# Another order of gatings, low parts and down products in a fused attention and feed-forward kernel

## The reference, cut to what matters

```python
xn = x / sqrt(mean(x * x) + 1e-6) * rms_g          # first layer
g = xn @ w_gate                                     # 512 -> 1536
val = xn @ w_val                                    # 512 -> 1536
x1 = (g * sigmoid(g) * val) @ w_out                 # 1536 -> 512
h = x1 @ w_in                                       # second layer, 512 -> 2048
y = (h * sigmoid(h)) @ w2_out                       # 2048 -> 512
```

## Time and profile before

| what | value |
|---|---|
| time, median of 3 (lowest to highest) | 916.54 us (915.85 to 919.73) |
| the profiled execution: time, span in the trace | 915.6 us, 913.9 us |
| mean granted clock of TensorE | 0.994 |
| busy: TensorE, VectorE, ScalarE, GpSimd | 884.3, 520.3, 343.7, 254.3 us |
| chain that ended last: TensorE, issue, GpSimd, VectorE | 85%, 4%, 4%, 4% of the span |

### The profile page before, as it was taken

How to read it: one execution, slowest core, us unless ns; L and a number is a source line. 1 busy time by engine, 2 the same in 40 slices (tenths; PEclk the granted TensorE clock), 3 DMA queues, 4 the chain that set the end, 5 groups by cost and what they waited for, 6 DMA issues and landing times.

```text
span 913.9 us, 12772 instructions
## 1 busy us (share of the span) xinstructions
PE 884.3 (97%) x4902; PEld 831.2 (91%) x4902; DVE 520.3 (57%) x865; ACT 343.7 (38%) x668; POOL 254.3 (28%) x266
## 2 busy tenths in 40 slices
PE   4898998999999999999999999999999999999998
PEld 4787898999999999999999999999999898889897
DVE  7788863777654666655655445666545544343433
ACT  2576844444222232354554232232233332332222
POOL 2776378888200000547775100000000000000000
PEclk9999998999999999999999999999999999999999
DMA  9843355776875555166759666555554545474321
GB/s 272 223 127 107 114 218 219 276 277 267 341 278 208 207 207 208 43 257 227 291 214 391 241 236 250 205 209 208 206 191 174 207 173 207 173 271 177 127 89 74
DMA packets 55724, 191.67 MB, mean 210 GB/s; under 512 B 21872, under 2 KB 32112, under 8 KB 42608
## 3 DMA queue, kind: packets, MB, share of 16 engines
q1 hardware_dynamic: 55664, 190.85, 58.0%
HBM read 134.74 MB, written 56.10 MB: 209 GB/s over the span
## 4 chain that ended last, share of the span: by engine, by line
PE 85%; issue 4%; POOL 4%; DVE 4%; DMA 2%; SPq 1%; ACT 1%; POOLq 0%; DVEq 0%; ACTq 0%
PE ps L1218 15%; PE ps L1219 14%; PE ps L1220 14%; PE ps L1282 7%; PE ps L1283 7%; PE ps L1281 7%; PE ps L1255 6%; PE ps L1256 6%; PE ps L1257 5%; PE ps L1152 1%; DMA qs<-in_q 1%; DVE al L990 1%; PE ps L1124 1%; DVE vt L983 1%; POOL rstd L568 1%
## 5 line engine op out<-in xcount | busy, mean ns | idle before, releaser
L1218 PE MATMUL ps<-xh,wr 128*128 128x384 f32 x840 | 282.6, 336 | 3.8 <-DVE qt L956 1.6
L1220 PE MATMUL ps<-xh,wr 128*128 128x384 f32 x840 | 281.1, 335 | 0.0
L1219 PE MATMUL ps<-xl,wr 128*128 128x384 f32 x840 | 280.9, 334 | 0.0
L1218 PEld LDWEIGHTS ps<-xh,wr 128*128 128x128 f32 x840 | 157.7, 188 | 8.3 <-DVE qt L956 2.5
L1219 PEld LDWEIGHTS ps<-xl,wr 128*128 128x128 f32 x840 | 157.7, 188 | 0.9
L1220 PEld LDWEIGHTS ps<-xh,wr 128*128 128x128 f32 x840 | 157.7, 188 | 0.0
L1283 PE MATMUL ps<-wo,al 128*128 128x512 f32 x288 | 112.5, 391 | 0.0
L1282 PE MATMUL ps<-wo,ah 128*128 128x512 f32 x288 | 112.4, 390 | 0.0
L1281 PE MATMUL ps<-wo,ah 128*128 128x512 f32 x288 | 112.0, 389 | 0.0
L1003 DVE TENSOR_TENSOR xacc<-ps,xacc 128x384 f32<-128x384 f32 (+1 forms) x102 | 62.4, 612 | 70.0 <-PE ps L1257 39.2
L1255 PE MATMUL ps<-ah,wo 128*128 128x384 f32 x288 | 97.8, 340 | 3.4 <-ACT qt L685 3.1
(11 more groups left out here) (128 smaller groups left out, 1171.8 us busy)
## 6 DMA issues: line engine op xcount, KB each, us to landing
wr<-ring_home SPq DMA_DIRECT2D x40, 1792.0 KB, 7.3
ring_home<-wr SPq DMA_DIRECT2D x20, 1792.0 KB, 8.1
wo<-out_home SPq DMA_DIRECT2D x28, 1024.0 KB, 4.8
out_home<-wo SPq DMA_DIRECT2D x14, 1024.0 KB, 9.6
raw_c<-in_moe_w_out SPq DMA_DIRECT2D x13, 512.0 KB, 7.3
qs<-in_q SPq DMA_DIRECT2D x16, 256.0 KB, 4.0
kv<-in_k SPq DMA_DIRECT2D x3, 1024.0 KB, 7.1
kv<-in_v SPq DMA_DIRECT2D x3, 1024.0 KB, 8.6
```

The costliest lines, as they stand in the source:

```text
L1218: pe.matmul(out_ps, w_hi, x_hi, start=first and c == 0, stop=False, skip_group_check=True)
L1219: pe.matmul(out_ps, w_hi, x_lo, start=False, stop=False, skip_group_check=True)
L1220: ins = pe.matmul(out_ps, w_lo, x_hi, start=False, stop=c == 1, skip_group_check=True)
```

## The change

Five edits, all in order and waits; no operation is added or left out.

1. The gatings have an order of their own, C11, C21, C12, C22, and the high and low parts of the first layer follow it. In the V unit run the first three gatings and low part 0, behind them; the gating of C22 runs in the following unit, between combine_u2 and combine_u3, and low parts 1, 2 and 3 after combine_u3. ScalarE makes one high part in the V unit and three in the following one.
2. A down of the first layer takes its products in the order perm 0, perm 1, rot 0, rot 1, perm 2, rot 2, rot 3, perm 3. It starts when two low parts are there and waits for all four at rot 0.
3. copy_down of a phase's last down moves out of that down's place in ScalarE's list into the unit behind it, after keep_first and the high parts. For the last down of all it stays.
4. In a down of the first layer the first of the token parts due there runs ahead of the first addition of a rot.
5. The waits follow: the overwriting of qt by keep_first, combine_u2 and combine_u3 waits for the gating that reads the same block, and banks BY and BZ are free after the second and third gating.

```diff
--- before.py
+++ after.py
@@ -113,10 +113,11 @@
                 (BX, 1, 1, False), (BY, 2, 6, False), (BZ, 6, 2, False)]
     C11, C12, C21, C22 = 0, 1, 2, 3
     SILUS = [C11, C22, C21, C12]
-    SPLITS = {1: [C11, C22, C21, C12], 2: [C11, C21, C22, C12]}
-
-
-    DOWN1 = [("rot", 0), ("rot", 1), ("perm", 0), ("perm", 1), ("rot", 2), ("rot", 3), ("perm", 2), ("perm", 3)]
+    GATES = [C11, C21, C12, C22]
+    SPLITS = {1: GATES, 2: [C11, C21, C22, C12]}
+
+
+    DOWN1 = [("perm", 0), ("perm", 1), ("rot", 0), ("rot", 1), ("perm", 2), ("rot", 2), ("rot", 3), ("perm", 3)]
     ROTBANK = [BR, BX, BR, BX]
 
 
@@ -660,7 +661,7 @@
                 if units[u][1] == "V":
                     gated = [m for m in range(n) if ffn_of[m] == 1]
                     if gated:
-                        act.wait_ge(s_lo, 4 * gated[-1] + 3)
+                        act.wait_ge(s_lo, 4 * gated[-1] + 2)
                     if downs[n] == (3, 0):
                         act.wait_ge(s_wlo, len(made))
                     if n == 0:
@@ -669,7 +670,7 @@
                     act.wait_ge(s_vb, B)
                     act.wait_ge(s_kTm, B)
                 elif ffn_of[n - 1] == 1:
-                    act.wait_ge(s_hd, hd0[n - 1] + 3)
+                    act.wait_ge(s_hd, hd0[n - 1] + 2)
                 else:
                     act.wait_ge(s_lo, 4 * (n - 1) + 2)
                 act.activation(tiles(u)[:, C21, :], ps[:, BX, 0:BLOCK], ACT.Copy).then_inc(s_snap, 1)
@@ -732,8 +733,12 @@
                     squares(NT - 1)
                     norm(NT - 1)
                 if prior == 1:
+                    high(n - 1, 1)
                     high(n - 1, 2)
                     high(n - 1, 3)
+                prev = before["unit", x]
+                if prev and prev[0] == "down" and prev[1] in last_down:
+                    copy_down(prev[1])
                 if x in (1, 2):
                     weight_high(made_at["r", x + 1] - (x == 2))
                 if x == 2:
@@ -750,7 +755,6 @@
                     weight_high(made_at["o", N2 + g])
                 if letter == "V":
                     high(n, 0)
-                    high(n, 1)
                 else:
                     silu(x, 0)
                     silu(x, 1)
@@ -810,8 +814,6 @@
                 if ph < 5:
                     for f in HIGH_AT[PHASES[ph][0]].get(g, ()):
                         token_high(ph + 1, f)
-                if x in last_down:
-                    copy_down(x)
                 if letter == "I":
                     high(n, 0)
                     high(n, 1)
@@ -948,7 +950,7 @@
                 if units[u][1] == "V" and gated:
                     dve.wait_ge(s_lo, 4 * gated[-1] + 4)
                 elif units[u][1] != "V" and n and ffn_of[n - 1] == 1:
-                    dve.wait_ge(s_hd, hd0[n])
+                    dve.wait_ge(s_hd, hd0[n - 1] + 3)
                 elif units[u][1] != "V" and n:
                     dve.wait_ge(s_lo, 4 * n)
                 dve.wait_ge(s_prod, NF * u + 2)
@@ -957,6 +959,9 @@
                    .then_inc(s_c, 1)
 
             def combine_u3(u):
+                n = units[u][3]
+                if units[u][1] != "V" and n and ffn_of[n - 1] == 1:
+                    dve.wait_ge(s_hd, hd0[n])
                 dve.wait_ge(s_prod, NF * u + 4)
                 dve.tensor_tensor(tiles(u)[:, C22, :], ps[:, BY, 0:BLOCK], tiles(u)[:, C21, :], ALU.add)\
                    .then_inc(s_c, 1)
@@ -973,12 +978,12 @@
                    .then_inc(s_c, 1)
 
             def gate(u, i):
-                n, c = units[u][3], SILUS[i]
-                dve.wait_ge(s_silu, 4 * n + i + 1)
+                n, c = units[u][3], GATES[i]
+                dve.wait_ge(s_silu, 4 * n + SILUS.index(c) + 1)
                 if c == C11:
                     dve.wait_ge(s_prod, NF * u + 5)
                 else:
-                    dve.wait_ge(s_c, 5 * u + 2 + i)
+                    dve.wait_ge(s_c, 5 * u + 2 + SILUS.index(c))
                 value = vt[:, c, :] if c == C22 else ps[:, {C11: BX, C21: BY, C12: BZ}[c], 0:BLOCK]
                 dve.tensor_tensor(vt[:, c, :], qt[:, c, :], value, ALU.mult).then_inc(s_hd, 1)
 
@@ -1012,21 +1017,21 @@
                 if x == 0:
                     scale_x(NT - 2)
                 if prior == 1:
-                    low(n - 1, 0)
-                    low(n - 1, 1)
+                    gate(x - 1, 3)
                 combine_u3(x)
                 if prior == 1:
+                    low(n - 1, 1)
                     low(n - 1, 2)
                     low(n - 1, 3)
                 if letter == "V":
                     gate(x, 0)
-                    gate(x, 1)
                 combine_last(x, C21)
                 if letter == "V":
-                    gate(x, 2)
+                    gate(x, 1)
                 combine_last(x, C12)
                 if letter == "V":
-                    gate(x, 3)
+                    gate(x, 2)
+                    low(n, 0)
 
             sum_keys(0, 0)
             dve.wait_ge(s_frontsum[0], 1)
@@ -1075,6 +1080,10 @@
                     letter = None
                     low(x, 2)
                     low(x, 3)
+                if ffn_of[x] == 1:
+                    for i in todo[:1]:
+                        token_part(ph + 1, i)
+                    todo = todo[1:]
                 add_down(x, 0)
                 add_down(x, 1)
                 for i in todo[:-1]:
@@ -1191,7 +1200,7 @@
                 elif i == 1 and u == 0:
                     pe.wait_ge(s_shift, NT)
                 elif i in (1, 2) and u and units[u - 1][1] == "V":
-                    pe.wait_ge(s_hd, hd0[units[u - 1][3]] + 2 + i)
+                    pe.wait_ge(s_hd, hd0[units[u - 1][3]] + 1 + i)
                 elif i in (1, 2) and u:
                     pe.wait_ge(s_c, 5 * u - 2 + i)
                 elif i == 3:
@@ -1235,8 +1244,10 @@
                 ph, g = downs[n]
                 w, ends = wo[o_slot(n)], (g == 0, g == GROUPS[1] - 1)
                 weights_of_down(n)
-                pe.wait_ge(s_lo, 4 * n + 4)
+                pe.wait_ge(s_lo, 4 * n + 2)
                 for kind, m in DOWN1:
+                    if kind == "rot" and m == 0:
+                        pe.wait_ge(s_lo, 4 * n + 4)
                     if kind == "rot" and m == 0 and n == 0:
                         pe.wait_ge(s_xc, NT)
                     elif kind == "rot" and m == 0:
```

## The result

| | before | changed |
|---|---|---|
| median of 6 runs (lowest to highest) | 916.53 us (915.85 to 919.73) | 909.34 us (907.92 to 912.24) |
| the profiled execution: time, span, mean granted clock | 915.6, 913.9, 0.994 | 909.0, 907.3, 0.998 |
| start of unit 0 in the trace | 111.71 us | 110.35 us |

The ratio is 0.9926 [0.9904, 0.9949]: 7.2 us faster, where 2.9 was forecast and 909.8 was the low end of the range.

What follows compares the result with a forecast made beforehand. TensorE was taken as the bound, busy 884.3 of 913.9 us, so only its waits could be won. Terms 0.5 + 0.35 + 2.0 + 0.86 + 0.4 - 1.2 = 2.9 us gave 913.6 us, range 909.8 to 917.3.

Steps and rivals of the forecast that it cites:

- First down: First layer's first down: silu chain 1.57 us late, five products left behind the wait instead of seven; gain 0.5 us.
- Unit 4: Unit 4: old stall at product 5 goes, product 3 stalls 0.7 us behind weight copies; gain 0.35 us.
- Units 6, 8, 10 and the down starts: Gating of C22 out of the V unit ends stalls at product 1, leaving 0.25 us each; gain 2.0 us.
- Rots later: Rots later in first-layer downs: banks free in time, slack 0.28 us; cost 0, at most 0.1 in each of 18.
- Unit 53: Unit 53, behind a phase's last down: copies of standing outputs moved a unit later remove its stall; gain 0.86 us.
- unit 45: Unit 45, behind a phase's last down: only the copy ahead of high 0 goes; gain 0.4 us.
- Unit 25: Unit 25: later load puts GpSimd's sums over the four low parts, 1.05 us each, not 0.47; loss 1.2 us.
- the lock of the earlier trace: VectorE and GpSimd on SBUF: VectorE's operation ends some 0.42 us after GpSimd's current one; GpSimd's next loses about 0.33.
- Weights pacing phase 0: Rival: TensorE waits again for GpSimd's weights for what it gains in phase 0; no gain, 916.5 us; chance 0.14.
- The clock was down for half as long: Rival on the first down: shorter wait keeps the clock at 2.4 GHz, 2.6 us more, 911.0 us; chance 0.12.
- No collisions: Rival: GpSimd's operations fall beside the moved ones in units 4 to 10 and 25; gain 6.1, 910.4 us; chance 0.17.
- The lock costing more than it gave: Rival: waits on GpSimd cost 2.0 us in each of units 4, 6, 8, 10; slower, 920.1 us; chance 0.09.

Runs made afterwards that it cites:

- experiment 5: The changed kernel as it is, in more executions: 912.71 us (8 runs), ratio 0.9959 against the kernel before.
- run 7: The kernel before with only ScalarE's copy of the first output weights moved from unit 2 into unit 1: 908.93 us, ratio 0.9930.
- run 6: The changed kernel with ScalarE's copy of the first output weights moved from unit 2 into unit 1: 905.47 us, ratio 0.9889 against the kernel before.
- run 2: The changed kernel with the copies of the standing outputs back in the last down's place: 913.31 us, ratio 0.9977 against the kernel before.
- run 3: The kernel before with only the down's new product order, its wait for three low parts and the token part moved ahead: 913.73 us, ratio 0.9976.
- run 4: The changed kernel with the old order of the down's products, all four low parts awaited at its start: 916.92 us, ratio 1.0016 against the kernel before.
- run 1: The kernel before with only the copies of the standing outputs moved a unit later: 914.61 us, ratio 0.9993.
- Run 8: The changed kernel with the raw tile's load in unit 24 also waiting for the second addition of down 11: 912.24 us, one execution.
- run 9: Changed kernel, first output weights' copy in unit 1, unit 3's high 0 ahead of its weight copies, second output weights' copy in unit 4: 905.77 us, ratio 0.9896.
- run 10: The changed kernel with low part 0 in the following unit, ahead of the moved gating: 912.59 us, one execution.

## Why the prediction was wrong

Point by point, in the order of the prediction.

**First down: +0.5, measured +1.54.** The chain came where it was put. The timeline of the changed kernel, from the copy to the product that waits:

```profile
130.35 1.04 ACT L622 ACTIVATE wo<-raw_f 128x1024 fp32r<-128x1024 f32 x1
...
131.47 1.29 POOL L552 TENSOR_TENSOR wo<-raw_f,wo 128x512 fp32r<-128x512 f32 x1 [5.13 <-ACT wo L622]
...
132.73 1.60 POOL L553 TENSOR_TENSOR wo<-raw_f,wo 128x512 fp32r<-128x512 f32 x1
...
137.12 0.73 POOL L533 TENSOR_TENSOR wt<-raw_g,wt 128x256 f32<-128x256 f32 x1
...
139.74 0.47 ACT L686 ACTIVATE qt<-ps 128x384 f32<-128x384 f32 x1
...
140.26 0.69 PE L1266 MATMUL ps<-ah,wo 128*128 128x384 f32 x1 [2.46 <-ACT qt L686]
```

Unit 2 began 1.67 us earlier than before (126.40, 128.07), so 1.67 is to be added to compare with before: the silu at 141.41 against 139.82 in the earlier trace rows, 1.59 later, where 1.57 was forecast. The first down began 0.54 us later than I had it. The forecast had it that it "needs low 1 only"; it waited for GpSimd's second low part of the output weights (line 553), which took 1.60 us instead of 1.28 beside the low parts of VectorE and ended at 134.33, with TensorE going on at 134.38. So the wait inside was 2.46 us and not 3.1. The half clock lasted 3.4 us instead of 6.8 (0.76 in the 7 us stretch, 0.51 before): the five products behind the wait took 6.86 us, 1.66 over their bare 5.2, where the forecast took over 2.6. That is 0.9 of the 1.0 us by which this term was too small; the bound of 3.4 us covered it. It leaves 0.6 for the order, near the 0.5 forecast.

**Unit 4: +0.35, measured -0.65.** Here as well the times were right: down 1 began at 163.42, which is 165.09 in the frame of before; the forecast's was 165.1. Only, the two terms aren't independent. The weights' chain sets when down 1 can start, so what the first down gives back early, unit 4 waits for. Product 3 of unit 4 starts 32.75 us behind the start of unit 2 in this profile and 32.70 in that of experiment 5, whose first down was 1.56 us shorter. Together they give 0.89, where 0.85 was forecast, and this agreement is luck: without half clock in either (runs 7 and 6) the two places give 0.36, and in experiment 5 down 1 starts 0.8 us later against unit 2 than before.

```profile
156.07 1.04 ACT L622 ACTIVATE wo<-raw_c 128x1024 fp32r<-128x1024 f32 x1
...
158.55 0.55 DVE L958 TENSOR_TENSOR qt<-ps,qt 128x384 f32<-128x384 f32 x1
...
159.15 0.44 PE L1227 MATMUL ps<-xh,wr 128*128 128x384 f32 x1 [1.44 <-DVE qt L958]
```

Product 3 waits 1.44 us for the combine (line 956 of before), in the place and for the engine that the prediction named, but for twice the 0.7 us given.

**Units 6, 8, 10 and the down starts: +2.0, measured +2.53.** Of the 0.25 us left on each, unit 6 has 0.27 and units 8 and 10 have 0.01 in this profile. In that of experiment 5 it is 0.00, 0.36 and 0.39, with the delay at product 3 as forecast, and the three units and the down starts give 2.05. So the 2.0 holds, and the 0.5 on top of it differs from execution to execution. Which edit does it I had wrong (runs 2, 3 and 4): the down's order gives 1.7 of it by itself.

**Rots later: 0, measured 0.** The downs take 8.32 us, and no unit behind one waits at product 0.

**Unit 53: +0.86, measured +0.84; unit 45: +0.4, measured +0.32.** Both hold, and runs 1 and 2 show that the copies alone do it.

**Unit 25: -1.2, measured +0.44. This is the step that failed**, 1.6 us of the 2.3 between 2.9 and 5.2 (0.32 without half clock, run 7 to run 6). "The sums move to 406.2 to 409.7, over the four low parts" took the load's time over unchanged. The timeline of the changed kernel, the load, GpSimd's first sum behind it, the first low part of unit 25 and the combine:

```profile
394.12 0.38 SPq L370 DMA_DIRECT2D raw_d<-in_moe_w_in  x1
...
397.80 0.74 POOL L528 TENSOR_TENSOR wt<-raw_d 128x256 f32<-128x256 f32 x1 [4.59 <-DMA raw_d<-in_moe_w_in]
...
401.84 0.56 DVE L995 TENSOR_TENSOR al<-qt,ah 128x384 fp32r<-128x384 f32 x1 [1.10 <-ACT ah L704]
...
403.84 0.56 DVE L958 TENSOR_TENSOR qt<-ps,qt 128x384 f32<-128x384 f32 x1
```

The load went out 1.6 us later against unit 24, as forecast. But the sum began 3.7 us behind it and not 6.9 (397.64 to 404.58 in the earlier trace rows). The sums are over before the low parts begin, a low part takes 0.56 us, and unit 25 gains the copy's 0.4. What differs stands in the view by tile, with the time from issue to landing. In the kernel before, the store of weights into the ring (1792 KB) and the load (512 KB):

```profile
L383 SPq DMA_DIRECT2D ring_home<-wr x1: 320/320/320, 391.3 to 391.3; - x1
...
DMA to landing us min/median/max: 8.6/8.6/8.6
```

```profile
L369 SPq DMA_DIRECT2D raw_d<-in_moe_w_in x1: 383/383/383, 397.6 to 397.6; - x1
...
DMA to landing us min/median/max: 6.8/6.8/6.8
```

In the changed kernel:

```profile
L384 SPq DMA_DIRECT2D ring_home<-wr x1: 319/319/319, 385.0 to 385.0; - x1
...
DMA to landing us min/median/max: 10.0/10.0/10.0
```

```profile
L370 SPq DMA_DIRECT2D raw_d<-in_moe_w_in x1: 383/383/383, 394.1 to 394.1; - x1
...
DMA to landing us min/median/max: 3.5/3.5/3.5
```

Before, the store landed at 399.9, 2.2 us behind the load's issue. In the changed kernel the store was issued 0.4 us ahead of unit 24's start (385.42) and not 0.8 us behind it (390.51), as GpSimd finished these weights earlier, and landed at 395.0, 0.9 us behind the load's issue. Run 8 bears this out from the other side: no DMA moved in the 4 us ahead of its load, which then landed in 3.7 us, though it went out later against unit 24 than in either kernel.

```profile
393.41:397.41 4.00, 4.00 (x25) 4.00 (x24) 2.45 (x5) 0.99 (x2) 0.00 (x0) 1.00 0.00 0
```

(The last column but one is the share of the DMA engines.) Two more transfers go out within 1 us of the load in each of the twelve profiles, so they aren't what differs.

The other profiles bound the cause. With load and store in their old places (before, runs 1 and 7) the store landed 2.2, 1.7 and 1.9 us behind the load's issue, and the load took 6.8, 4.8 and 5.8 us. In the eight where the store landed at most 0.9 us behind it (the changed kernel, runs 2 to 6, 9 and 10), the load took 3.5 to 4.3. In run 3 the load is nearly at its old place, 7.4 us behind unit 24's start against 7.1, and only the store went out 1.2 us earlier: 3.7 us. So the longer load goes with the store's end and not with the load's own place. But 6.8 was the longest of three in the same place, so it was a number of one execution too. In run 1, with both in their old places, unit 25 already takes 7.70 us.

**Unit 1: none, measured +0.31; unit 15: none, +0.28.** In unit 1 the gating of C22 lay over GpSimd's last low part, for which unit 2 waits. That gating and the low part in the timeline before, then the low part in the changed kernel:

```profile
125.92 0.94 DVE L983 TENSOR_TENSOR vt<-qt,vt 128x384 f32<-128x384 f32 x1
...
126.40 1.61 POOL L545 TENSOR_TENSOR wr<-wt,wr 128x512 fp32r<-128x512 f32 x1
```

```profile
125.05 1.30 POOL L546 TENSOR_TENSOR wr<-wt,wr 128x512 fp32r<-128x512 f32 x1
```

This is the lock of the earlier trace rows seen from GpSimd's side, where I had only asked what VectorE loses. Each profile with the new gatings has 7.85 to 7.87 us there, each with the old ones 8.17 to 8.19. Unit 15 goes with the gatings in the same way (7.28 to 7.31, 7.57 to 7.59). There product 3 comes late: the combine that it waits for starts 2.69 us into the unit before and 2.35 in the changed kernel, behind an idle VectorE. Why is open.

**The rivals.** Weights pacing phase 0 is what happened between the first down and unit 4 and nowhere else. The clock was down for half as long. No collisions came nearest, in unit 25, in units 8 and 10 of the first profile, and in its time, 910.4; this last is luck in part, as the change is worth 4.5 us and not the 6.1 of that rival. The lock costing more than it gave isn't what the change shows. Nearest to it come unit 4 (9.01 us instead of 8.36) and run 10.

**The range** ended at 909.8 and missed by 0.5 us. The mechanisms would have been inside it: 4.5 us of change put the time at 912.0. So unit 25 explains why the gain was larger than 2.9, and not by itself why the time left the range. What the range lacked was a term for where the clock falls in a set of six runs (the 916.54 of the runs shown was taken as fixed). Against the medians of the last row of the table above, the six of before lay 1.0 us high and the six of the changed kernel 1.7 low.

## What to carry to other kernels

When a transfer's issue is moved, look up what it shares the DMA engines with at the new place: the time that a load took beside a store is no property of the load. Follow a chain of weights or hidden parts to the next point where it gates TensorE, and take the time gained ahead of that point off what is gained behind it. And where a kernel's first wait in a down is due to the place of a single copy, move the copy: that gave more here (nearly 7 us) than the reordering around it. And before a few us between two sets of runs are put on a change, compare executions with the same mean granted clock, and repeat the profile: a wait read from one execution can be another's by some tenths of a us.

## What the runs showed of the hardware

- The same wait of 2.5 us of TensorE was followed by 3.4 us at half clock in one execution of the changed kernel and by none in another, and between executions of one program at a mean granted clock of 0.998 and those at 0.994 lie 2.2 us (before) and 3.3 (changed).
- A 512 KB load landed 4.8 to 6.8 us behind its issue where a 1792 KB store took 1.7 to 2.2 us more to land (three profiles), 3.5 to 4.3 where the store took at most 0.9 (eight), and 3.7 where none was under way (run 8).
- Where VectorE and GpSimd both work on SBUF alone, both lose: run 8's low parts took 0.89 to 1.10 us instead of 0.56, and in unit 1 of the kernel before a GpSimd operation took 1.61 us, 1.30 in the changed kernel.
